# Feed-forward of a tile pair spread over 21 steps of two blocks, in a fused attention and gated-convolution kernel

## What is computed

```
scores = z @ z.T / S                 # z: S x 64, S = 3136
x = u * (max(scores, 0) ** 2 @ v)    # u, v: S x 256
h = max(x @ w_in, 0)                 # w_in: 256 x 1024
c[s] = conv_w[0]*h[s-1] + conv_w[1]*h[s] + conv_w[2]*h[s+1]
out = (h * sigmoid(c)) @ w_out       # w_out: 1024 x 256
```

## Time and profile before

| | us |
|---|---|
| median of 3 runs | 1936.87 |
| lowest, highest | 1934.24, 1938.0 |
| the profiled execution | 1933.92 |
| its span, first to last instruction | 1932.1 |
| PE busy in it | 1710.3 (89%) |
| DVE busy | 1379.7 (71%) |
| ACT busy | 1188.2 (61%) |
| POOL busy | 133.2 (7%) |

### The profile page before, as it was taken

One profiled execution on the slowest core, in us unless ns is written; L12 is line 12 of the kernel. 1 busy time (PEld: TensorE's weight loads), 2 busy tenths in 40 slices (PEclk: granted clock), 3 DMA queues, 4 the chain that ended last, 5 costly groups with the idle time before them and its releaser, 6 DMA issues.

```text
span 1932.1 us, 37660 instructions
## 1 busy us (share of the span) xinstructions
PE 1710.3 (89%) x15600; PEld 1539.1 (80%) x15600; DVE 1379.7 (71%) x1825; ACT 1188.2 (61%) x2010; POOL 133.2 (7%) x106
## 2 busy tenths in 40 slices
PE   7889998987988999898899989899888998999896
PEld 6778887877888888787788878788777887888785
DVE  6577668667676777767777686767778667776875
ACT  7556656665665666566566566656766655665664
POOL 4100000022000000002200000000320000000000
PEclk9999999998998999899999999989999999999998
DMA  4100000121000000012100000010210000000000
GB/s 124 40 25 1 25 25 16 32 63 42 11 25 25 1 25 25 15 33 68 45 1 25 25 15 11 25 47 1 70 44 15 11 25 25 1 25 25 11 11 20
DMA packets 26426, 53.16 MB, mean 28 GB/s; under 512 B 2704, under 2 KB 13456, under 8 KB 26256
## 3 DMA queue, kind: packets, MB, share of 16 engines
q1 hardware_dynamic: 26256, 50.76, 8.2%
HBM read 37.89 MB, written 12.85 MB: 26 GB/s over the span
## 4 chain that ended last, share of the span: by engine, by line
PE 59%; DVE 27%; ACT 8%; issue 4%; DMA 1%; POOL 0%; ACTq 0%; SPq 0%
PE ps_av L317 24%; PE ps_y L358 14%; PE ps_s L298 10%; PE ps_h L339 10%; DVE attn L614 7%; DVE g_sb L644 7%; DVE g_lo L664 6%; DVE attn_lo L621 4%; ACT attn L473 3%; ACT attn_hi L482 2%; DVE x_sb L629 2%; ACT g_sb L516 1%; DVE g_sb L658 1%; ACT g_sb L522 1%; DVE g_sb L652 1%
## 5 line engine op out<-in xcount | busy, mean ns | idle before, releaser
L473 ACT ACTIVATE attn<-ps_s 128x448 f32<-128x448 f32 x700 | 344.8, 543 | 622.8 <-PE ps_s L298 595.2
L317 PE MATMUL ps_av<-attn_lo,v_hi 64*128 64x448 f32 x2744 | 563.8, 370 | 42.2 <-DVE x_sb L629 42.2
L614 DVE SCALAR_TENSOR_TENSOR attn<-ps_s,attn 128x448 f32<-128x448 f32 x700 | 404.9, 618 | 262.2 <-ACT attn L473 261.5
L621 DVE TENSOR_TENSOR attn_lo<-attn,attn_hi 128x896 fp32r<-128x896 f32 (+1 forms) x364 | 392.8, 1079 | 251.5 <-ACT attn_hi L482 250.4
L317 PE MATMUL ps_av<-attn_hi,v_hi 64*128 64x448 f32 x2744 | 558.7, 366 | 0.0
L317 PE MATMUL ps_av<-attn_hi,v_lo 64*128 64x448 f32 x2744 | 557.1, 365 | 0.0
L317 PEld LDWEIGHTS ps_av<-attn_lo,v_hi 64*128 64x128 f32 x2744 | 308.2, 189 | 71.7 <-issue 52.0
L482 ACT ACTIVATE attn_hi<-attn 128x896 fp32r<-128x896 f32 (+1 forms) x364 | 335.1, 921 | 27.5 <-DVE attn L614 25.3
L317 PEld LDWEIGHTS ps_av<-attn_hi,v_hi 64*128 64x128 f32 x2744 | 308.6, 189 | 17.7
L358 PE MATMUL ps_y<-g_hi,w_hi 64*128 64x448 f32 (+1 forms) x856 | 194.0, 414 | 141.8 <-DVE g_lo L664 141.8
L317 PEld LDWEIGHTS ps_av<-attn_hi,v_lo 64*128 64x128 f32 x2744 | 306.4, 188 | 15.6
(11 more groups left out here) (49 smaller groups left out, 1642.5 us busy)
## 6 DMA issues: line engine op xcount, KB each, us to landing
u_sb<-u_win SPq DMA_DIRECT2D x28, 448.0 KB, 3.3
raw<-v_all SPq DMA_DIRECT2D x48, 256.0 KB, 2.7
out<-y_sb SPq DMA_DIRECT2D x24, 448.0 KB, 3.4
z_raw<-z_win SPq DMA_DIRECT2D x28, 224.0 KB, 3.5
raw<-z_all SPq DMA_DIRECT2D x12, 256.0 KB, 3.7
w_raw<-w_all SPq DMA_DIRECT2D x8, 256.0 KB, 2.8
out<-y_sb SPq DMA_DIRECT2D x4, 450.0 KB, 2.6
raw<-v_all SPq DMA_DIRECT2D x4, 128.0 KB, 2.3
```

The source lines that it names most:

```text
L317: done = mm(ps_av[:, c, 0:BLOCK], v[rows, j * MODEL + c * P:j * MODEL + (c + 1) * P], a[rows, 2 * slot(n, p) + e, :], start=p == 0 and not ...
L473: act.activation(attn[:, slot(n, p), e, :], ps_s[:, e, 0:BLOCK], ACT.Relu, scale=1.0 / SEQ / SEQ).then_inc(relu_ready, 1)
L614: dve.scalar_tensor_tensor(a, ps_s[:, e, 0:BLOCK], 0.0, a, ALU.max, ALU.mult).then_inc(attn_ready, 1)
L621: dve.tensor_tensor(attn_lo[:, at:at + k, :], attn[:, slot(n, p), 0:k, :], attn_hi[:, at:at + k, :].bitcast(F32), ALU.subtract).then_inc(a ...
```

## The change

The chain of a pair F is spread over more steps. Steps s count from the start of the block behind m and go up to 20: s = 13 to 20 are steps 0 to 7 of the block after that, so that two blocks' feed-forward is in flight (`in_flight`, `due`). Both halves of a down projection are in the same step, the first ahead of the scores, the second behind `attend`. `round_x` and `split_x` move to the end of the block. On ACT and DVE the attention work of a step goes ahead of the feed-forward, with `relu_scores` ahead of `round_attn` and `multiply` ahead of `split_attn`, and the feed-forward goes in the order from the latest link to the earliest. `copy_y` is at s = 20, and PE waits for it (`y_ready`) before the first down of the next block. SP stores y behind the piece loads of a closing block. In the steps behind the last block, `feed` finishes block 26: its downs of F = 2 and 3 now stand there, at t = 3 and 6.

```diff
@@ -78,16 +78,16 @@
-UP_FIRST = {1: 0, 3: 1, 5: 2}
-UP_SECOND = {2: 0, 4: 1, 6: 2}
-DOWN_FIRST = {7: 0, 9: 1, 11: 2}
-DOWN_SECOND = {8: 0, 10: 1, 12: 2}
-UP_FIRST_END = {7: 3}
-UP_SECOND_END = {8: 3}
-RELU_AT = {3: 0, 5: 1, 7: 2, 9: 3}
-TAP01_AT = {4: 0, 6: 1, 8: 2, 10: 3}
-GATE_AT = {5: 0, 7: 1, 9: 2, 11: 3}
-SPLIT_AT = {6: 0, 8: 1, 10: 2, 12: 3}
+UP_FIRST = {1: 0, 4: 1, 7: 2, 10: 3}
+UP_SECOND = {2: 0, 5: 1, 8: 2, 11: 3}
+TAP0_AT = {3: 0, 6: 1, 9: 2, 12: 3}
+TAP1_AT = {3: 0, 6: 1, 9: 2, 14: 3}
+TAP2_AT = {5: 0, 8: 1, 9: 2, 15: 3}
+GATE_AT = {6: 0, 9: 1, 10: 2, 16: 3}
+ROUND_G_AT = {7: 0, 10: 1, 14: 2, 17: 3}
+DOWN_AT = {9: 0, 12: 1, 16: 2, 19: 3}
+COPY_Y_AT = 20
+LONGEST = 21
 WINDOW_AT = 6
...
@@ -219,6 +219,14 @@
...
+        def in_flight(n, p):
+            return [(n - 1 - k, p + k * PAIRS) for k in range(2) if n - 1 - k >= 0 and p + k * PAIRS < LONGEST]
+        def due(n, p, table):
+            return [(m, table[s]) for m, s in in_flight(n, p) if m < BLOCKS - 1 and s in table]
         block = ctx.enter_context(nc.Block())
@@ -249,11 +257,11 @@
...
                     sp.dma_start(z_raw[:, :], z_win[n + 1]).then_inc(z_loaded, 16)
-                if n > 1:
-                    store(n - 2)
                 if more:
...
                         load_piece(b + 1, g)
+                if n > 1:
+                    store(n - 2)
...
@@ -350,6 +358,8 @@
...
                         pe.wait_ge(down_done, 2 * (m * FP + F))
+                    if m > 0 and F == 0:
+                        pe.wait_ge(y_ready, m)
                 turn = int(second)
...
@@ -379,6 +389,8 @@
...
                 pe.wait_ge(down_done, 2 * (m * FP + F))
+                if F == 0:
+                    pe.wait_ge(y_ready, m)
                 for e in range(2):
...
@@ -390,45 +402,32 @@
...
-                m = n - 1
-                if p == 0 and n > 1:
-                    down_half(n - 2, FP - 1, False)
-                if n > 0 and p in UP_FIRST:
-                    up_half(m, UP_FIRST[p], False)
-                if n > 0 and p in UP_SECOND:
-                    up_half(m, UP_SECOND[p], True)
-                if n > 0 and p in DOWN_FIRST:
-                    down_half(m, DOWN_FIRST[p], False)
-                if n > 0 and p in DOWN_SECOND:
-                    down_half(m, DOWN_SECOND[p], True)
+                for m, F in due(n, p, UP_FIRST):
+                    up_half(m, F, False)
+                for m, F in due(n, p, UP_SECOND):
+                    up_half(m, F, True)
+                for m, F in due(n, p, DOWN_AT):
+                    down_half(m, F, False)
...
-                m = n - 1
-                if p == 0 and n > 1:
-                    down_half(n - 2, FP - 1, True)
-                if n > 0 and p in UP_FIRST_END:
-                    up_half(m, UP_FIRST_END[p], False)
-                if n > 0 and p in UP_SECOND_END:
-                    up_half(m, UP_SECOND_END[p], True)
+                for m, F in due(n, p, DOWN_AT):
+                    down_half(m, F, True)
...
                 for p in range(PAIRS):
-                    if p == LAST:
-                        attend(n, p, False)
-                        middle(n, p)
-                    else:
-                        attend(n, p, False)
-                        middle(n, p)
+                    attend(n, p, False)
+                    middle(n, p)
                     if ahead_of(n, p, AHEAD):
...
                     end(n, p)
-            down(BLOCKS - 2, FP - 1)
             for t in range(STEPS_ALONE):
+                for m, F in due(BLOCKS, t, DOWN_AT):
+                    down(m, F)
                 for f in range(FT):
...
@@ -534,28 +533,32 @@
...
+            def feed(n, p):
+                for m, F in due(n, p, ROUND_G_AT):
+                    round_gated(m, F)
+                for m, F in due(n, p, GATE_AT):
+                    gate(m, F)
+                for m, F in due(n, p, TAP0_AT):
+                    first_tap(m, 2 * F)
+                    first_tap(m, 2 * F + 1)
+                for m, F in due(n, p, UP_SECOND):
+                    relu_h(m, 2 * F, False)
+                    relu_h(m, 2 * F + 1, False)
+                for m, s in in_flight(n, p):
+                    if s == COPY_Y_AT:
+                        copy_y(m)
             def step(n, p):
-                m = n - 1
-                if n > 0 and p == 0:
-                    round_x(m)
-                if n > 1 and p == 1:
-                    copy_y(n - 2)
-                if n > 0 and p in RELU_AT:
-                    for f in (2 * RELU_AT[p], 2 * RELU_AT[p] + 1):
-                        relu_h(m, f, False)
-                if n > 0 and p in TAP01_AT:
-                    for f in (2 * TAP01_AT[p], 2 * TAP01_AT[p] + 1):
-                        first_tap(m, f)
+                if ahead_of(n, p, AHEAD):
+                    relu_scores(*ahead_of(n, p, AHEAD))
+                if p == LAST:
+                    round_x(n)
                 if ahead_of(n, p, AHEAD - 1):
                     round_attn(*ahead_of(n, p, AHEAD - 1))
-                if ahead_of(n, p, AHEAD):
-                    relu_scores(*ahead_of(n, p, AHEAD))
+                feed(n, p)
                 if p == WINDOW_AT and n + 1 < BLOCKS:
                     split_window(n + 1)
-                if n > 0 and p in GATE_AT:
-                    gate(m, GATE_AT[p])
-                if n > 0 and p in SPLIT_AT:
-                    round_gated(m, SPLIT_AT[p])
                 if n == 0:
...
@@ -586,13 +589,11 @@
...
             for t in range(STEPS_ALONE):
-                if t == 0:
-                    round_x(m)
                 for f in range(FT):
...
                         relu_h(m, f, True)
-                if t == START_ALONE[0] + 3:
-                    copy_y(m - 1)
+                if t < PAIRS:
+                    feed(BLOCKS, t)
                 for f in range(FT):
...
@@ -664,24 +665,27 @@
...
+            def feed(n, p):
+                for m, F in due(n, p, ROUND_G_AT):
+                    split_gated(m, F)
+                for m, F in due(n, p, GATE_AT):
+                    apply_gate(m, F)
+                for m, F in due(n, p, TAP1_AT):
+                    convolve(m, F)
+                for m, F in due(n, p, TAP2_AT):
+                    convolve_last(m, F)
             def step(n, p):
-                m = n - 1
-                if n > 0 and p in GATE_AT:
-                    convolve_last(m, GATE_AT[p])
-                if ahead_of(n, p, AHEAD - 1):
-                    split_attn(*ahead_of(n, p, AHEAD - 1))
-                if n > 0 and p == 0:
-                    split_x(m)
                 if p == LAST:
...
                     multiply(*ahead_of(n, p, AHEAD))
-                if n > 0 and p in TAP01_AT:
-                    convolve(m, TAP01_AT[p])
-                if n > 0 and p in GATE_AT:
-                    apply_gate(m, GATE_AT[p])
-                if n > 0 and p in SPLIT_AT:
-                    split_gated(m, SPLIT_AT[p])
+                if ahead_of(n, p, AHEAD - 1):
+                    split_attn(*ahead_of(n, p, AHEAD - 1))
+                if p == LAST:
+                    split_x(n)
+                feed(n, p)
...
```

## The result

The changed kernel takes 1642.12 us (median of 4 runs, 1640.62 to 1642.21), the kernel before 1935.55 in the runs beside it: a ratio of 0.8487, 95% interval 0.8464 to 0.8511. Forecast were 1658 and a range of 1632 to 1740.

A forecast was written before the change was run, and what follows sets the result against it. Order and hand-offs between engines were taken as the bound. Block 0 62.3, block 1 52, normal blocks 1249, closing 189, block 27 55.1 and tail 46 gave 1653.4 of span, 1655.2 executed, 1658 as median; range 1632 to 1740 us.

The forecast's parts named there:

- What bounds: Whole kernel: order and hand-offs bound it; PE work is 56.6 us of a 66.40 us block, at 0.2016 us a pair.
- item 4: Down projections: split_gated two or more steps, at least 7 us, ahead of its down; the 141.8 us of waits vanish.
- item 5: Block start: gate_by_u done 1.2 us after attend(12), covered by 3.0 us of PE work; the 42.2 us of waits go.
- item 3: Scores and split_attn hand-offs: room 0.55 us at step 12, 0.5 at step 0, 0.3 for split_attn(1); the tightest points.
- rival (a): Block boundary: late split_attn leaves a residual stall of 1 to 4 us per block, 1739 us; chance 0.18.
- item 6: Added y_ready wait before the first down: over 4 us of room for copy_y, price 0.
- item 7: Three closing blocks: POOL work delays DVE, which becomes the bound; 63 us each taken, between 57 and 72.7.
- item 8: Block 0: multiply first opens a loop of 3.48 us a step; 65.3 becomes 62.3 us (bounds 59 to 66).
- Block 1: Second block, without downs of a block before it: 256.5 pairs, 51.7, say 52 us.
- Block 27 and tail: Last block without scores at its end, 273 pairs, 55.1 us; tail with one more down, 46 us (44 to 50).
- Normal blocks: Blocks 2 to 26 without the closing ones: 22 x 56.6 = 1245 us, plus 0.2 each for hand-offs, 1249.
- Rival (c): All steps: a result PE wants before its next scores closes a loop, 77 us a block, 2190 us; chance 0.05.

The follow-up runs named there:

- the order alone: Kernel before with its old step tables, only the order inside a step changed on ACT and DVE (most of the new order): 2289.93 us, 1.185 times the kernel before.
- the empty step 11: Changed kernel with four edits, among them tap 2 of pair 2 moved from step 9 to 11: 1659.48 us against 1647.06 for the changed kernel on the same chip.
- the feed-forward first: Changed kernel with all feed-forward ahead of attention on ACT and DVE, round_attn ahead of relu_scores, split_attn ahead of multiply: 1744.14 us.
- x in step 0: Changed kernel with round_x and split_x moved back to step 0 of the next block: 1749.84 us.

## Why the prediction was right

- *What bounds.* The price of a pair of matmuls from the undisturbed stretch gave 56.6 us a block; 56.60 is what it is. This term carried the sum.
- *Downs (item 4).* Right: the waits are gone, and one step less of distance brings 7.2 us a block of them back. The method, time after the scores' end against PE's interval, also gave the size of the waits it was tried on, within 0.3 us. But "at least 7 us" was no room: it counts from the scores of step 7 and leaves out what DVE does behind them. In block 12 `copy_y`, `split_gated` and the down that wants both stand so:

```profile
721.40 0.92 ACT L534 ACTIVATE y_sb<-ps_y 128x896 f32<-128x896 f32 x1
721.71 1.08 DVE L665 TENSOR_TENSOR g_lo<-g_sb,g_hi 128x896 fp32r<-128x896 f32 x1
725.25 0.39 PE L368 MATMUL ps_y<-g_hi,w_hi 64*128 64x448 f32 x2
```

`split_gated` is done 2.5 us ahead of the down. One step of 4.2 us less makes that a wait of 1.7, and 1.62 and 1.66 were measured.
- *Block start (item 5).* Right that the wait goes, wrong in the room: 3.0 us of PE work cover `gate_by_u`, 1.8 don't, and 1.2 us less of cover cost 0.82, so the room was 0.4 us and not 1.8. The end of block 11 shows the step that was wrong, that `gate_by_u` starts with the end of `attend(12)`:

```profile
681.68 0.36 PE L325 MATMUL ps_av<-attn_hi,v_lo 64*128 64x448 f32 x1
682.16 1.09 DVE L622 TENSOR_TENSOR attn_lo<-attn,attn_hi 128x896 fp32r<-128x896 f32 x1
683.17 1.15 DVE L630 TENSOR_TENSOR x_sb<-ps_av,u_sb 128x448 f32<-128x448 f32 x2
684.65 0.36 PE L325 MATMUL ps_av<-attn_lo,v_hi 64*128 64x448 f32 x1
```

The last attend matmul ends at 682.04, but `split_attn` of step 11 stands ahead on DVE, and `gate_by_u` starts 1.1 us later. It was luck that 0.4 was left.
- *Rooms (item 3).* The place was right (step 12), and rival (a), given 0.18, didn't come, but by a hair: 0.56 us more in step 12 cost 0.55.
- *y_ready (item 6).* Price 0, right; the room is 2.9 us (`copy_y` ends at 722.32 in the rows above), not over 4, and one step later costs a wait of 1.5 us a block.
- *Closing blocks (item 7).* Mis-sized: 63 taken, 59.83 measured (59.8 to 61.9 in all runs of this kernel). DVE is the bound there, as said, and its loss did grow, from 7 to 9.3 us. But a normal block leaves DVE 8.3 us idle (56.60 against 48.34), and 6 of the 9.3 us went into that; 3.2 reached the length. 9.5 us of the miss in the sum.
- *Block 0 (item 8).* 62.3 against 60.20, right in kind: between 20 and 42 us `multiply` comes every 3.0 to 3.3 us, where it came every 3.2 to 3.7.
- *Block 1.* 52 against 53.80: it has the one `x_sb` wait of 1.4 us that is left, and a clock of 0.94.
- *Block 27 and tail.* 55.1 against 54.38, 46 against 47.59.
- *Normal blocks.* 22 x 56.8 against 22 x 56.59: the 0.2 us for hand-offs was not needed, 4 us.

Together -2.1 + 1.8 - 4.1 - 9.5 - 0.7 + 1.6 = -13.0 us, the 13 us between the summed span of 1653.4 and 1640.4. The other 2.8 us to the forecast of 1658 were added because the median had been 0.15% above the profiled execution before; here the two are 1642.12 and 1642.19.

Rival (c) had a low chance, and didn't come; the order alone, at 80.2 us a block where (c) gave 77, showed that such a loop is real and dear.

## What to carry to other kernels

With several in-order engines, write down for each step when a result is ready and when the next engine wants it, both from one common event (here the end of the scores), and give each link of a long side chain a step to spare. An edit of such a table must be followed to the first thing of the next step too: each of my misses (`copy_y` a step later, a tap in the empty step 11, `round_x` ahead of `round_attn`) was work whose follower I had not looked at. And room is to be counted from the end of the work that stands ahead on the same engine, and not from the step number: two rooms of this prediction, 7 and 1.8 us, were 2.5 and 0.4. A change made of tables and of orders can't be judged by its halves either: most of one half alone cost 18% here, the other brought two thirds.

## What the runs showed of the hardware

- *A stall costs more than the idle that is shown.* 0.61 us of idle lengthened a block by 0.82, 0.33 by 0.55, 1.50 + 0.61 by 2.60 to 2.67, 7.20 in four waits by 8.35, and 2.25 in five, with the feed-forward first, by 3.56: 0.2 to 0.3 us on top of each. Two parts of it show at the wait of the earlier trace rows: the pair at 715.71 is followed by the next at 716.02, 0.31 us later instead of 0.20, and the shown idle starts only at the modelled end of the last matmul, 0.37 us behind its start, where pairs are else 0.20 apart.
- *The clock after a stall.* Normal blocks with waits of 1.50 and 0.61 us kept a granted clock of 1.00. Blocks with one wait of 2.54 us (x in step 0) had 0.97 mostly and 1.00 in some, and were 1.75 us apart; blocks with a wait of 2.26 and three of 1.6 to 1.7 us were of both kinds, too (66.5 and 64.95 us). The same stall can be followed by the lower level or not.
- *Closing blocks of one kernel differ.* In the repeated run of the changed kernel they took 61.92, 59.82 and 61.92 us. DVE was busy 2.1 us longer in the long ones (59.68 against 57.58) with the same work, and PE's scores waits were 2.7 us instead of 1.8. Why the loss to POOL differs was not found.
